# Windowed attention and two dense layers: the loads of later attention heads issued by SyncE, between the weight loads, instead of by GpSimd

## The chip, the cores and the metric

The kernel runs on one core of a Trainium2 chip. What is measured is the device time of one execution in microseconds (us); lower is better. The core's engines run side by side, each through its own list of instructions in order: TensorE (PE in the profile), VectorE (DVE), ScalarE (ACT), GpSimd (POOL) and SyncE (SP). They wait for each other by semaphores. DMA transfers are issued by an engine's list (here SyncE and GpSimd) and then run by themselves; a semaphore is raised when one has landed.

## The reference

Two batches of 8 heads, 768 positions, head dimension 64. Attention is limited to the last 128 positions and the first 4 (sinks). Its output, 1536 tokens of 512 features, goes through two dense layers of width 2048.

```python
scores = scale * np.matmul(q, k.transpose(0, 1, 3, 2))
keep = is_sink | in_window                 # pos < 4, or 0 <= rel < 128
scores = np.where(keep, scores, -1000000000.0)
a = np.exp(scores - np.max(scores, axis=-1, keepdims=True))
a = a / (np.sum(a, axis=-1, keepdims=True) + 1e-09)
x = np.matmul(a, v)                        # then heads side by side: 1536 x 512

h = x @ w_in                               # layer 1: 512 -> 2048
g = np.where(h >= 1, h, np.where(h <= -1, 0.0, (h + 1) ** 2 / 4))
x = g @ w_out                              # 2048 -> 512

h = x @ w_in2                              # layer 2
g = np.where(h > 0.0, h, np.exp(np.minimum(h, 0.0)) - 1.0)
y = g @ w_out2
```

All inputs are float32.

## The kernel before

The tokens are cut into six chunks of 256. Layer 1 runs over them one by one, and beside layer 1 of a chunk the kernel computes the attention of the next chunk; only chunk 0's attention stands alone, at the start (`first_...`). Layer 2 then runs over three chunks of 512 tokens. To keep precision, every operand of the dense layers is split in two parts, `_hi` (a rounding that TensorE multiplies fast, made by ScalarE) and `_lo` (the rest, made by VectorE by a subtraction), and each product is three matmuls (lines 507 to 509 and 522 to 524). The keys and queries of a head are split likewise (`split_head`, lines 593, 594 on ScalarE, 782, 783 on VectorE).

A layer's chunk has 16 steps t, one per 128 of the 2048 hidden features. A step of TensorE is `hidden(t)` (12 matmuls into `h_ps`), `outward(t - 2)` (12 matmuls) and, beside them, parts of the attention of the next chunk: `attention_plan` puts the scores of heads 0 to 7 at steps 2, 3, 5, 6, 8, 9, 11, 12, a head's exponentials one step later, its transposes two steps later, and a pair's values three steps after its second head. A head h > 0 is split at the head of its own step (`before_layer`), head 0 between two chunks.

The weights come in groups of 512 KB, 16 for a layer (`load_weights`, line 290). During layer 1 of chunk 0 they are split too: groups 0 to 2 before it, group 3 + t at the end of step t (`splits_first`; ScalarE line 644, VectorE line 840). A weight group is loaded into one of six buffers: groups 0 to 4 take the first five, group 5 + n takes buffer n mod 6. A load therefore waits (line 284) until the group that had its buffer has been split: group 5 until group 0 has, ..., group 9 until group 4 has, group 10 takes a new buffer once the first attention is over, group 11 waits for group 5, ..., group 15 for group 9. SyncE issues these loads in a fixed order written out by hand (lines 292 to 318), then the stores of the result.

The loads for the attention of chunks 1 to 5 are issued by GpSimd (`load_head`, `load_values`, lines 370 to 388, called from line 394 on). The keys of a head (260 KB, `ks`) and its queries (128 KB, `qs`) go into one of two buffers, by the parity of the head; a load waits until the head before the last has been split by VectorE (`qk_lo_ready`). Heads 0 and 1 of chunk 1 wait for the first chunk's scores instead. The values of a pair of heads (192 KB and 36 KB, `vals`) go into one of two buffers, and wait until the pair before the last has been used (`attn_ready`; for the first two, `first_attn`). GpSimd also builds the masks at the start and copies the mask of each chunk (line 409).

What sets the order of the work is thus the list of each engine; an engine that waits in its list holds up all that stands behind it.

Of the kernel before, what the change touches and what calls it, by code (L numbers as in the profile page):

```python
# [30 lines left out]
B, HEADS, SEQ, HD = 2, 8, 768, 64  # L31
# [3 lines left out]
NC = TOK // CT  # L35
# [4 lines left out]
PAIRS = HEADS // 2  # L40
# [5 lines left out]
NW = 2 * GROUPS  # L46
# [35 lines left out]
def build(nc, qk_first, v_first, q_t, k_t, v_w, v_s, w_in, w_out, ident_d, out, n_sink, window):  # L82
# [6 lines left out]
    KS = 2 * LOW + 2 * NS  # L89

    with ExitStack() as ctx:
# [6 lines left out]
        def sem(name):  # L98
            return ctx.enter_context(nc.semaphore(name))
# [24 lines left out]
        qs, ks = sb0("qs", [P, 2, CT]), sb0("ks", [P, 2, QB * SW])  # L124
# [3 lines left out]
        vs = vals[:, 0:6 * P].rearrange("p (s b d) -> p s b d", s=2, b=3)  # L128
        vsink = vals[:, 6 * P:8 * P].rearrange("p (s d) -> p s d", s=2)
# [21 lines left out]
        first_scores, first_max, first_neg_max, first_exp = sem("first_scores"), sem("first_max"), sem("first_neg_max"), sem("first_exp")  # L151
        first_sum, first_inv, first_probs, first_probs_t = sem("first_sum"), sem("first_inv"), sem("first_probs"), sem("first_probs_t")
        first_copied, first_attn = sem("first_copied"), sem("first_attn")
        qk_loaded = [sem(f"qk_loaded{n}") for n in range(4)]
        v_loaded = [sem("v_loaded0"), sem("v_loaded1")]
# [46 lines left out]
        def heads_before(c, h=0):  # L202
            return (c - 1) * HEADS + h

        def pairs_before(c, p=0):
            return (c - 1) * PAIRS + p
# [64 lines left out]
        @block.sync  # L271
        def _(sp):
            def load_first_head_pair(p):
                sp.dma_start(first_qk[p][0], qk_first[p, :, 0, :]).then_inc(first_qk_loaded[p], 16)
                sp.dma_start(first_qk[p][1], qk_first[p, :, 1, :]).then_inc(first_qk_loaded[p], 16)

            def load_first_values(p):
                sp.dma_start(first_v[p], v_first[p]).then_inc(first_v_loaded[p], 16)

            def load_weights(i):  # L280
                n = order[i]
                layer, m = n // NW, n % NW
                if splits_until_free(i) > 0:
                    sp.wait_ge(w_lo_ready, splits_until_free(i))
                if i < NW and place[i] >= FEW:
                    sp.wait_ge(first_attn, PAIRS)
                if i >= NW:
                    sp.wait_ge(attn_ready, pairs_before(NC))
                src = (w_in if m % 2 == 0 else w_out)[layer, m // 2]
                sp.dma_start(raw_buffer(i), src).then_inc(raw_loaded[place[i]], 16)  # L290

            load_first_head_pair(0)
            load_first_head_pair(1)
            sp.dma_start(ident[:, :], ident_d).then_inc(ident_loaded, 16)
            load_first_values(0)
            load_first_head_pair(2)
            load_first_values(1)
            load_weights(0)
            load_first_head_pair(3)
            load_first_values(2)  # L300
            load_first_values(3)
            load_weights(1)
            load_weights(2)
            load_weights(3)
            load_weights(4)
            load_weights(5)
            load_weights(6)
            load_weights(7)
            load_weights(8)
            load_weights(9)  # L310
            load_weights(10)
            load_weights(11)
            load_weights(12)
            load_weights(13)
            load_weights(14)
            load_weights(15)
            for i in range(NW, 2 * NW):
                load_weights(i)
            with sp.Fori(0, NC1) as c:
                for m in range(KT):  # L320

                    sp.wait_ge(y_written, NC * len(y_ps) + (c * KT + (m + 1)))
                    sp.dma_start(out[:, m, bass.ts(c, CT1)], chunk(c, 1)[:, m, :]).then_inc(stored, 16)
            sp.wait_ge(stored, 16 * NC1 * KT)


        @block.gpsimd
        def _(pool):
            steps = [0]

            def step(ins):
                steps[0] += 1
                ins.then_inc(mask_step, 1)
                pool.wait_ge(mask_step, steps[0])

            def keep_where(view, base, pattern, channel):
                step(nc.gpsimd.affine_select(out=view, in_=view, compare_op=ALU.is_ge, fill=MASKED / SCALE,
                                             base=base, pattern=pattern, channel_multiplier=channel))

            def build_mask(m, kind):  # L340

                step(nc.gpsimd.memset(m, 0.0))
                for j in range(QB):
                    start = j * MW + NS
                    prev, own = m[:, start:start + P], m[:, start + P:start + WIN]
                    if kind == 0 and j == 0:
                        step(nc.gpsimd.memset(prev, MASKED / SCALE))
                    else:

                        keep_where(prev, window - 1 - P, [[1, P]], -1)  # L350

                    keep_where(own, 0, [[-1, P]], 1)
                    if window < P:
                        keep_where(own, window - 1, [[1, P]], -1)
                    if kind == 0:
                        step(nc.gpsimd.memset((own if j == 0 else prev)[:, 0:NS], MASKED / SCALE))

            def build_first_mask(m):

                step(nc.gpsimd.memset(m, 0.0))  # L360
                own0, prev1, own1 = (m[:, n * P:(n + 1) * P] for n in range(3))
                for own in (own0, own1):
                    keep_where(own, 0, [[-1, P]], 1)
                    if window < P:
                        keep_where(own, window - 1, [[1, P]], -1)
                keep_where(prev1, window - 1 - P, [[1, P]], -1)
                for sinks in (own0, prev1):
                    step(nc.gpsimd.memset(sinks[:, 0:NS], 0.0))

            def load_head(c, h):  # L370
                if isinstance(c, int) and c == 1 and h < 2:

                    pool.wait_ge(first_scores, h + 2)
                else:
                    pool.wait_ge(qk_lo_ready, heads_before(c, h) - 1)
                for to, src in zip((ks[:, h % 2, :], qs[:, h % 2, :]), (k_t, q_t)):
                    pool.dma_start(to, src[bass.ds(heads_before(c, h), 1)].rearrange("o p n -> (o p) n")).then_inc(qk_loaded[h % 4], 16)  # L377

            def load_values(c, p):
                s = p % 2  # L380
                if isinstance(c, int) and c == 1 and p < 2:
                    pool.wait_ge(first_attn, PAIRS - 1)
                else:
                    pool.wait_ge(attn_ready, pairs_before(c, p) - 1)
                n = pairs_before(c, p)
                pool.dma_start(vs[:, s, :, :].rearrange("p b d -> p (b d)"),
                             v_w[bass.ds(n, 1)].rearrange("o p n -> (o p) n")).then_inc(v_loaded[s], 16)
                pool.dma_start(vsink[0:KS, s, :], v_s[bass.ds(n, 1)].rearrange("o p n -> (o p) n")).then_inc(v_loaded[s], 16)

            build_first_mask(mask[:, 0:SEEN])  # L390
            pool.sem_inc(mask_ready, 1)
            build_mask(masks[:, 0, :], 0)
            build_mask(masks[:, 1, :], 1)
            load_head(1, 0)
            load_head(1, 1)
            pool.wait_ge(first_max, HEADS * QB)
            nc.gpsimd.tensor_copy(mask[:, :], masks[:, 1, :]).then_inc(mask_ready, 1)
            load_values(1, 0)
            load_values(1, 1)
            for h in range(2, HEADS):  # L400
                load_head(1, h)
                if h > 2 * 2 and h % 2 == 1:
                    load_values(1, h // 2)
            with pool.Fori(2, NC) as c:
                load_head(c, 0)
                load_head(c, 1)
                pool.wait_ge(max_done, heads_before(c) * QB)
                kind = (c % CPB + (CPB - 1)) // CPB
                nc.gpsimd.tensor_copy(mask[:, :], masks[:, bass.ds(kind, 1), :].rearrange("p o n -> p (o n)")).then_inc(mask_ready, 1)
                for p in range(PAIRS):  # L410
                    if p > 0:
                        load_head(c, 2 * p)
                        load_head(c, 2 * p + 1)
                    load_values(c, p)


        @block.tensor
# [563 lines left out]
```

## Time and profile before

| | us |
|---|---|
| median of 3 runs (lowest, highest) | 656.87 (655.11, 657.06) |
| the profiled execution | 657.06 |
| its span, first to last instruction | 655.4 |
| TensorE busy | 635.3 |
| VectorE busy | 378.3 |
| ScalarE busy | 350.0 |
| GpSimd busy | 74.3 |

The profile records one execution. The span is shorter than the time by 1.7 us, which lie before the first and after the last instruction. Matmuls overlap in TensorE's pipeline, so its busy time says how much of the span it has something under way, not how fast it works. A wait in a list of waits is the idle time of an engine ahead of an instruction, with the engine or transfer that ended it. The time of a DMA transfer "to landing" is counted from its issue.

### The profile page before, as it was taken

How to read it: one execution, taken by the hardware profiler on the slowest of the kernel's cores; microseconds unless marked ns; L12 is line 12 of the kernel's file. 1: busy time of each engine (PE TensorE's matmuls, PEld its weight loads, DVE VectorE, ACT ScalarE, POOL GpSimd, SP SyncE). 2: the span in 40 equal slices, each digit the busy share in tenths (PEclk: the TensorE clock that was granted, in tenths of full speed). 3: DMA queues.
4: the chain of work that ended last, by engine and by line, in shares of the span. 5: the costliest groups of instructions: out<-in, count | busy, mean ns of one | idle time of the engine just before them, and what ended most of it. 6: DMA issues, size and time to landing. Idle time of an engine off the chain costs nothing.

```text
span 655.4 us, 12200 instructions
## 1 busy us (share of the span) xinstructions
PE 635.3 (97%) x4164; PEld 562.6 (86%) x4164; DVE 378.3 (58%) x994; ACT 350.0 (53%) x830; POOL 74.3 (11%) x147
## 2 busy tenths in 40 slices
PE   5789999999999999999999999999999999999997
PEld 3688889999999999999999988888888888888886
DVE  6799968886886788588757863322332222322221
ACT  5687756665665666566656563333443333533333
POOL 4111221320322122123000000000000000000000
PEclk9799999999999999999999999999999999999999
DMA  7674212320322222122044600000100000100001
GB/s 277 188 221 143 69 39 85 91 77 24 100 65 63 62 66 86 38 77 86 25 161 161 188 7 0 1 0 1 49 16 0 0 0 0 64 0 0 0 0 64
DMA packets 15275, 42.48 MB, mean 65 GB/s; under 512 B 2852, under 2 KB 4536, under 8 KB 15248
## 3 DMA queue, kind: packets, MB, share of 16 engines
q0 software_dynamic: 7040, 20.57, 10.7%
q1 hardware_dynamic: 8208, 21.56, 9.8%
q8 instruction: 15, 0.25, 0.2%
q14 instruction: 12, 0.10, 0.0%
HBM read 38.98 MB, written 3.15 MB: 64 GB/s over the span
## 4 chain that ended last, share of the span: by engine, by line
PE 88%; DVE 9%; ACT 1%; issue 1%; DMA 0%; ACTq 0%; SPq 0%; DVEq 0%
PE h_ps L507 13%; PE h_ps L509 13%; PE h_ps L508 13%; PE y_ps L522 10%; PE y_ps L524 9%; PE y_ps L523 9%; PE s_ps L524 3%; PE s_ps L523 3%; PE s_ps L522 3%; PE o_ps L490 3%; PE t_ps L470 2%; DVE wout_lo L840 1%; PE s_ps L461 1%; PE s_ps L460 1%; DVE win_lo L840 1%
## 5 line engine op out<-in xcount | busy, mean ns | idle before, releaser
L507 PE MATMUL h_ps<-x_hi,win_hi 128*128 128x256 f32 (+1 forms) x576 | 186.9, 324 | 0.4
L509 PE MATMUL h_ps<-x_hi,win_lo 128*128 128x256 f32 (+1 forms) x576 | 185.2, 321 | 0.0
L508 PE MATMUL h_ps<-x_lo,win_hi 128*128 128x256 f32 (+1 forms) x576 | 184.2, 320 | 0.0
L522 PE MATMUL y_ps<-g_hi,wout_hi 128*128 128x256 f32 (+1 forms) x480 | 147.1, 306 | 1.7 <-DVE g_lo L853 1.6
L524 PE MATMUL y_ps<-g_hi,wout_lo 128*128 128x256 f32 (+1 forms) x480 | 146.4, 305 | 0.0
L523 PE MATMUL y_ps<-g_lo,wout_hi 128*128 128x256 f32 (+1 forms) x480 | 145.9, 304 | 0.0
L870 DVE SCALAR_TENSOR_TENSOR g_full<-g_full,h_ps 128x512 f32<-128x512 f32 x48 | 33.1, 690 | 156.6 <-ACT g_full L675 156.6
L507 PEld LDWEIGHTS h_ps<-x_hi,win_hi 128*128 128x128 f32 x576 | 108.7, 189 | 10.6 <-DVE g_full L866 1.0
L508 PEld LDWEIGHTS h_ps<-x_lo,win_hi 128*128 128x128 f32 x576 | 109.2, 190 | 9.4
L509 PEld LDWEIGHTS h_ps<-x_hi,win_lo 128*128 128x128 f32 x576 | 108.9, 189 | 8.3
L662 ACT CAST g_hi<-g_full 128x256 fp32r<-128x256 f32 (+1 forms) x144 | 68.5, 476 | 68.6 <-DVE g_full L870 34.2
L853 DVE TENSOR_TENSOR g_lo<-g_full,g_hi 128x256 fp32r<-128x256 f32 (+1 forms) x144 | 73.7, 512 | 51.5 <-ACT g_hi L662 50.8
L522 PEld LDWEIGHTS y_ps<-g_hi,wout_hi 128*128 128x128 f32 x480 | 90.1, 188 | 7.8 <-issue 2.0
L523 PEld LDWEIGHTS y_ps<-g_lo,wout_hi 128*128 128x128 f32 x480 | 90.6, 189 | 4.7
L524 PEld LDWEIGHTS y_ps<-g_hi,wout_lo 128*128 128x128 f32 x480 | 90.4, 188 | 4.2
L673 ACT ACTIVATE ramp<-h_ps 128x512 f32<-128x512 f32 x48 | 28.8, 600 | 121.9 <-PE h_ps L509 121.8
L603 ACT ACTIVATE probs<-s_ps,small 128x260 f32<-128x260 f32 x80 | 37.4, 471 | 27.2 <-DVE small L798 27.1
L670 ACT ACTIVATE ramp<-h_ps,small 128x256 f32<-128x256 f32 x96 | 45.6, 475 | 7.7 <-PE h_ps L509 7.7
L864 DVE SCALAR_TENSOR_TENSOR g_full<-ramp 128x256 f32<-128x256 f32 x96 | 40.4, 421 | 10.6 <-ACT ramp L670 10.6
L377 POOL DMA_DIRECT2D ks<-in_k x40 | 22.1, 552 | 215.2 <-DVE q_parts L783 213.4
L866 DVE TENSOR_TENSOR g_full<-g_full,h_ps 128x256 f32<-128x256 f32 x96 | 40.4, 421 | 3.3
L524 PE MATMUL s_ps<-g_hi,wout_lo 128*128 128x512 f32 x96 | 38.3, 399 | 0.0
(109 smaller groups left out, 819.2 us busy)
## 6 DMA issues: line engine op xcount, KB each, us to landing
ks<-in_k POOLq DMA_DIRECT2D x40, 260.0 KB, 3.0
raw<-in_w_in SPq DMA_DIRECT2D x11, 512.0 KB, 4.3
raw<-in_w_out SPq DMA_DIRECT2D x11, 512.0 KB, 3.5
qs<-in_q POOLq DMA_DIRECT2D x40, 128.0 KB, 2.8
vals<-in_v POOLq DMA_DIRECT2D x20, 192.0 KB, 3.1
out_y<-xy SPq DMA_DIRECT2D x12, 256.0 KB, 2.1
xy<-in_w_in SPq DMA_DIRECT2D x5, 512.0 KB, 4.9
xy<-in_w_out SPq DMA_DIRECT2D x5, 512.0 KB, 4.0
```

The costliest lines, as they stand in the source:

```text
L507: pe.matmul(o, win_hi[:, k, f], x_hi[:, k, :], start=(k == 0), stop=False)
L508: pe.matmul(o, win_hi[:, k, f], x_lo[:, k, :], start=False, stop=False)
L509: last = pe.matmul(o, win_lo[:, k, f], x_hi[:, k, :], start=False, stop=(k == KT - 1))
L522: pe.matmul(o, wout_hi[:, t, cols], g_hi[:, t % GR, :], start=begin, stop=False, skip_group_check=True)
L523: pe.matmul(o, wout_hi[:, t, cols], g_lo[:, t % GR, :], start=False, stop=False, skip_group_check=True)
L524: last = pe.matmul(o, wout_lo[:, t, cols], g_hi[:, t % GR, :], start=False, stop=(t == FT - 1), skip_group_check=True)
L603: nc.scalar.activation(probs[:, j, hh * SW:(hh + 1) * SW], s_ps[j][:, 0:SW], ACT.Exp, bias=top[:, hh, j:j + 1], accum_out=total[:, hh, j:j ...
L662: nc.scalar.copy(g_hi[:, t % GR, :], g_full[:, t % 2, :]).then_inc(g_hi_ready, 1)
L670: nc.scalar.activation(ramp[:, t % 2, :], h, ACT.Relu, bias=half[:, 0:1], scale=0.5).then_inc(ramp_ready, 1)
L853: nc.vector.tensor_tensor(g_lo[:, t % GR, :], g_full[:, t % 2, :], g_hi[:, t % GR, :].bitcast(F32), ALU.subtract).then_inc(g_lo_ready, 1)
L864: nc.vector.scalar_tensor_tensor(g, r, 1.0, r, ALU.min, ALU.mult).then_inc(bent_ready, 1)
L866: nc.vector.tensor_tensor(g, g, h, ALU.max).then_inc(g_ready, 1)
```

## The change

The functions `load_head` and `load_values` move from GpSimd to SyncE, unchanged but for the engine that waits and issues. On SyncE the loads of chunk 1 are put between the weight loads by hand: heads 0 and 1 and the first values behind group 4, head 2 behind group 6, head 3 and the second values behind group 8, and heads 4 to 7 with their values behind group 15, the last of layer 1. Chunks 2 to 5 follow in a loop, then the weights of layer 2 as before. GpSimd keeps the masks and their copies. 120 transfers (40 of keys, 40 of queries, 40 for values) change the engine that issues them; none is added or removed, and their sizes are the same.

```diff
--- before.py
+++ after.py
@@ def _(sp):
+            def load_head(c, h):
+                if isinstance(c, int) and c == 1 and h < 2:
+                    sp.wait_ge(first_scores, h + 2)
+                else:
+                    sp.wait_ge(qk_lo_ready, heads_before(c, h) - 1)
+                for to, src in zip((ks[:, h % 2, :], qs[:, h % 2, :]), (k_t, q_t)):
+                    sp.dma_start(to, src[bass.ds(heads_before(c, h), 1)].rearrange("o p n -> (o p) n")).then_inc(qk_loaded[h % 4], 16)
+
+            def load_values(c, p):
+                s = p % 2
+                if isinstance(c, int) and c == 1 and p < 2:
+                    sp.wait_ge(first_attn, PAIRS - 1)
+                else:
+                    sp.wait_ge(attn_ready, pairs_before(c, p) - 1)
...
+
+            def load_pair(c, p):
+                load_head(c, 2 * p)
+                load_head(c, 2 * p + 1)
+                load_values(c, p)
...
             load_weights(4)
+            load_head(1, 0)
+            load_head(1, 1)
+            load_values(1, 0)
             load_weights(5)
             load_weights(6)
+            load_head(1, 2)
             load_weights(7)
             load_weights(8)
+            load_head(1, 3)
+            load_values(1, 1)
             load_weights(9)
-            load_weights(10)
...
-            load_weights(15)
+            for i in range(10, NW):
+                load_weights(i)
+            load_pair(1, 2)
+            load_pair(1, 3)
+            with sp.Fori(2, NC) as c:
+                for p in range(PAIRS):
+                    load_pair(c, p)
             for i in range(NW, 2 * NW):
                 load_weights(i)
@@ def _(pool):
-            def load_head(c, h):
...
             build_mask(masks[:, 1, :], 1)
-            load_head(1, 0)
-            load_head(1, 1)
             pool.wait_ge(first_max, HEADS * QB)
             nc.gpsimd.tensor_copy(mask[:, :], masks[:, 1, :]).then_inc(mask_ready, 1)
-            load_values(1, 0)
-            load_values(1, 1)
-            for h in range(2, HEADS):
-                load_head(1, h)
-                if h > 2 * 2 and h % 2 == 1:
-                    load_values(1, h // 2)
             with pool.Fori(2, NC) as c:
-                load_head(c, 0)
-                load_head(c, 1)
+
                 pool.wait_ge(max_done, heads_before(c) * QB)
                 kind = (c % CPB + (CPB - 1)) // CPB
                 nc.gpsimd.tensor_copy(mask[:, :], masks[:, bass.ds(kind, 1), :].rearrange("p o n -> p (o n)")).then_inc(mask_ready, 1)
-                for p in range(PAIRS):
-                    if p > 0:
-                        load_head(c, 2 * p)
-                        load_head(c, 2 * p + 1)
-                    load_values(c, p)
```

## Rows read from the trace of the kernel before

**Rows 1.** The page: busy us (share of span) xinstructions.

```profile
PE 635.3 (97%) x4164; PEld 562.6 (86%) x4164; DVE 378.3 (58%) x994; ACT 350.0 (53%) x830; POOL 74.3 (11%) x147
```

**Rows 2.** Stretches: length; busy us PE, PEld, DVE, ACT, POOL; granted clock; DMA share, GB/s.

```profile
60.00:84.50 24.50, 22.73 (x186) 20.95 (x187) 23.60 (x66) 18.36 (x49) 7.21 (x12) 1.00 0.26 76
...
96.00:150.00 54.00, 53.96 (x460) 52.23 (x459) 43.05 (x139) 34.82 (x101) 13.64 (x25) 1.00 0.27 78
```

**Rows 3.** Waits: who waited for whom, us in total, times, longest.

```profile
POOL ks L377 <- DVE q_parts L783: 213.4, 38, 12.7
...
PE o_ps L450 <- issue: 1.9, 1, 1.9
```

**Rows 4.** ScalarE in order of time: start us, length, line, operation.

```profile
26.11 0.63 ACT L593 CAST k_hi<-ks 128x520 fp32r<-128x520 f32 x1
...
33.03 1.04 ACT L644 CAST wout_hi<-raw 128x1024 fp32r<-128x1024 f32 x1
...
51.69 1.05 ACT L644 CAST wout_hi<-xy 128x1024 fp32r<-128x1024 f32 x1
...
57.78 0.65 ACT L593 CAST k_hi<-ks 128x520 fp32r<-128x520 f32 x1
```

**Rows 5.** GpSimd in order of time, its loads; in brackets the wait.

```profile
22.04 0.54 POOL L386 DMA_DIRECT2D vals<-in_v  x1 [6.24 <-PE o_ps L450]
...
28.51 0.54 POOL L377 DMA_DIRECT2D ks<-in_k  x1 [4.33 <-DVE q_parts L783]
...
38.04 0.62 POOL L377 DMA_DIRECT2D ks<-in_k  x1 [8.46 <-DVE q_parts L783]
...
46.58 0.54 POOL L377 DMA_DIRECT2D ks<-in_k  x1 [7.40 <-DVE q_parts L783]
```

**Rows 6.** SyncE in order of time, weight groups 9, 10 and 15.

```profile
33.48 0.34 SPq L290 DMA_DIRECT2D xy<-in_w_out  x1
...
33.86 0.43 SPq L290 DMA_DIRECT2D xy<-in_w_in  x1
...
55.91 0.34 SPq L290 DMA_DIRECT2D xy<-in_w_out  x1
```

**Rows 7.** DMA issues at 33.8 and 56 us, and the start's: KB, us to landing.

```profile
xy<-in_w_out SPq DMA_DIRECT2D x1, 512.0 KB, 4.0
...
xy<-in_w_in SPq DMA_DIRECT2D x1, 512.0 KB, 4.9
...
xy<-in_w_out SPq DMA_DIRECT2D x1, 512.0 KB, 3.3
...
ks<-in_qk_first SPq DMA_DIRECT2D x4, 128.0 KB, 2.4
```

**Rows 8.** VectorE in order of time, heads 0 and 4.

```profile
27.08 0.70 DVE L782 TENSOR_TENSOR k_lo<-ks,k_hi 128x520 fp32r<-128x520 f32 x1 [0.41 <-ACT q_parts L594]
...
59.08 0.69 DVE L782 TENSOR_TENSOR k_lo<-ks,k_hi 128x520 fp32r<-128x520 f32 x1
```

**Rows 9.** TensorE in order of time, near 60 and 86 us.

```profile
60.27 0.39 PE L460 MATMUL s_ps<-k_hi,q_parts 128*128 128x260 f32 x1 [0.59 <-DVE q_parts L783]
...
85.58 0.36 PE L522 MATMUL y_ps<-g_hi,wout_hi 128*128 128x256 f32 x1 [0.60 <-DVE g_lo L853]
```

**Rows 10.** VectorE's line 782, all heads: ns min/median/max.

```profile
L782 DVE TENSOR_TENSOR k_lo<-ks,k_hi x40: 692/700/703, 27.1 to 319.2; 128x520 fp32r<-128x520 f32 x40
```

**Rows 11.** Stretches around the fall of the clock, as in rows 2.

```profile
14.42:21.24 6.82, 3.48 (x32) 2.46 (x30) 5.43 (x19) 5.67 (x16) 0.62 (x1) 1.00 0.74 273
...
21.24:28.07 6.83, 5.82 (x31) 4.44 (x28) 4.13 (x10) 3.48 (x7) 2.14 (x4) 0.50 0.72 221
...
55.38:62.20 6.82, 6.00 (x49) 5.52 (x48) 6.64 (x18) 6.70 (x16) 1.07 (x2) 1.00 0.35 105
```

**Rows 12.** Chain of waits near 27 and 92 us: start us, us, what.

```profile
26.75 0.21 PE h_ps L507
...
92.11 0.12 PE y_ps L522
```

More of the change, by code:

```diff
@@ L278, in load_first_values @@
                 sp.dma_start(first_v[p], v_first[p]).then_inc(first_v_loaded[p], 16)
+            def load_head(c, h):
[11 more added lines that the diff above has]
+                    sp.wait_ge(attn_ready, pairs_before(c, p) - 1)
+                n = pairs_before(c, p)
+                sp.dma_start(vs[:, s, :, :].rearrange("p b d -> p (b d)"),
+                             v_w[bass.ds(n, 1)].rearrange("o p n -> (o p) n")).then_inc(v_loaded[s], 16)
+                sp.dma_start(vsink[0:KS, s, :], v_s[bass.ds(n, 1)].rearrange("o p n -> (o p) n")).then_inc(v_loaded[s], 16)
+            def load_pair(c, p):
+                load_head(c, 2 * p)
+                load_head(c, 2 * p + 1)
+                load_values(c, p)
             def load_weights(i):
@@ L305, in _ @@
             load_weights(4)
+            load_head(1, 0)
+            load_head(1, 1)
+            load_values(1, 0)
             load_weights(5)
             load_weights(6)
+            load_head(1, 2)
             load_weights(7)
             load_weights(8)
+            load_head(1, 3)
+            load_values(1, 1)
             load_weights(9)
-            load_weights(10)
[L312 to L315, printed above, removed]
-            load_weights(15)
+            for i in range(10, NW):
[5 more added lines that the diff above has]
+                    load_pair(c, p)
             for i in range(NW, 2 * NW):
@@ L368, in build_first_mask @@
                     step(nc.gpsimd.memset(sinks[:, 0:NS], 0.0))
-            def load_head(c, h):
[L371 to L388, printed above, removed]
             build_first_mask(mask[:, 0:SEEN])
```

## The prediction

> **What bounds the kernel now.** I read the page first, then the busy time by stretches, then who waits for whom. On the page TensorE is busy for 635.3 us of the span of 655.4 us [rows 1]. The stretches divide this in two. From about 96 us on TensorE has no holes (53.96 us busy of 54.00); the attention of the later chunks and both layers run at its pace, and what another engine or queue does there costs nothing as long as it keeps up. In chunk 0 (25 to 86 us) it is VectorE that has none: 23.60 us busy of 24.50 between 60.00 and 84.50 us, TensorE 22.73 [rows 2]. That chunk splits one weight group per step beside its attention. So a stop of VectorE there moves everything behind it, and later stages have no spare time in which to catch up.
>
> The waits say who needed the loads that are moved. GpSimd stood 213.4 us at the head loads, waiting for VectorE to free a head's buffer [rows 3]; in the whole list of waits nobody waits for one of these loads to land. They are hidden everywhere today, so the move can only gain if GpSimd's issuing harms somebody, and can lose wherever SyncE's order is later than GpSimd's.
>
> **The change, part by part.** I work through SyncE's new order with the times at which each wait ends today.
>
> Heads 0 and 1 of chunk 1: issued behind weight group 4, at about 9.5 and 11 us, behind 2.5 MB of weights (6.4 us at the rate worked out below), and head 0 is taken by ScalarE at 26.11 us [rows 4]. Nothing.
>
> Weight group 5 now stands behind the first values, whose wait ends at 22.04 us [rows 5]: it is issued at 23.0 us and, at the 4.9 us that is the longest landing used below, there at 27.9 us; ScalarE casts it at 33.03 us [rows 4]. Group 6 follows at 23.4 us and is cast later still. Group 7 stands behind head 2, whose wait ends at 28.51 us [rows 5]; two issues of 0.45 us put it at 29.4 us, and it is cast two steps after group 5; a step of chunk 0 is some 60/16 = 3.8 us. Hidden.
>
> Group 9 (33.48 us) now stands behind head 3, whose wait ends at 38.04 us [rows 5, 6], and behind two issues for it and two for values: 38.04 + 4 x 0.45 = 39.9 us. Groups 10 and 11 follow at 40.3 and 40.8 us, group 12 is where it was. Head 3, these values and the four groups are 2.66 MB in a row; at the rate worked out below (512 KB in 1.28 us) that is 6.7 us, over by 47 us, and group 9, the first of the groups, is cast at 51.69 us [rows 4]. Hidden.
>
> Head 4 is the one that isn't. Today its wait (head 2 split) ends at 46.58 us [rows 5] and GpSimd issues it at once, 11.2 us before ScalarE takes it at 57.78 us [rows 4]. After the change it stands behind weight groups 10 to 15, and group 15 waits until group 9 has been split: it is issued at 55.91 us [rows 6]. Head 4's keys are then issued at 55.91 + 0.34 + 0.04 = 56.3 us and its queries at 56.75 us. Now the landing. Group 15 lands 3.3 us after its issue [rows 7], at 59.2 us. Groups 9 and 10, issued back to back at 33.48 and 33.86 us, landed 4.0 and 4.9 us later [rows 6, 7], at 37.48 and 38.76 us: the second 512 KB took 1.28 us behind the first. So 260 KB of keys and 128 KB of queries behind group 15 take 0.65 + 0.32 us, and head 4 has landed at 60.2 us.
>
> There the Trainium skill has a rule (DMA: Bandwidth & Descriptors, "Queues, rings and completion order"): one issuing engine's transfers are consumed in ring order, while a GpSimd row is taken in turn with it, packet by packet. The landings of groups 9 and 10 [rows 7] agree with it: the later one has its 1.28 us to itself. Were SyncE's transfers shared out instead, head 4 could land near 59.1 us and the cost below would be some 1.1 us smaller.
>
> From landing to VectorE: ScalarE casts keys and queries, and VectorE started on head 0's keys 0.97 us after ScalarE did (26.11 to 27.08 us) [rows 4, 8]. So VectorE can start head 4 at 60.2 + 0.97 = 61.2 us. Today it starts at 59.08 us, straight from group 10's split with no idle time [rows 8]. It now stands still for 2.1 us. ScalarE's other work of the step (the cast of g and the ramp of step 8) comes behind the head's casts in its order and is late by as much. TensorE waited for VectorE's q_parts at 60.27 us already (0.59 us idle), and at 85.58 us for g_lo [rows 9]: it has no work in hand that could fill the hole, and VectorE no idle time before 85.6 us that could take it back. The 2.1 us go through to the end.
>
> What I take the 2.1 us from, and its bounds: at best, head 4's queries land like the 128 KB loads of the start, 2.4 us from their issue [rows 7], at 59.15 us; VectorE starts at 60.1 us and loses 1.0 us. At worst they take what group 10 took, 4.9 us, and land at 61.65 us: a loss of 3.5 us. The middle way is nearest to what follows a 512 KB transfer in this queue, so I keep 2.1.
>
> Head 5 is issued at 57.2 us, lands by 61.2 (0.97 us behind head 4) and is cast a step (3.8 us) later than head 4. The values of pair 2 follow at 58 us and are used three steps on. From here SyncE has caught up with VectorE: heads 6 and 7 and all of chunks 2 to 5 wait for the same semaphores in the same order as on GpSimd, with the same lead (a head is freed three steps before its successor is split). An issue takes 0.43 us on SyncE instead of 0.54 us on GpSimd; nobody waits for either. The second layer's weights waited for the last attention anyway.
>
> What GpSimd loses: 120 issues. What remains is the mask copy, whose waits don't change. If these issues disturbed VectorE, its instructions would differ in length where they meet. The split of the keys takes 692 to 703 ns over all 40 heads [rows 10]. I take nothing for it; what it would be worth if the harm lay in the gaps between them is rival C.
>
> Sum, against the profiled execution: 657.06 + 2.1 = 659.2 us (span 657.5). The median of the runs shown, 656.87, lies 0.2 us below that execution: 659.0. I take 659.1. That is 0.33% slower; I count 0.3% (2.0 us) as what a measurement of this kernel can tell from no change, so this forecast sits right on that bound.
>
> **Rivals.**
> A. The stall takes the clock with it. In chunk 0's beginning TensorE, busy 3.48 of 6.82 us, was followed by 6.83 us at a granted clock of 0.50 (1.2 GHz) [rows 11]. With the stall it would stand idle 2.1 + 0.6 us in one piece, in a stretch of which it now works 6.00 of 6.82 us. In the slow stretch a matmul follows the last after 0.21 us, at full clock after 0.12 us [rows 12]; 6.8 us at that pace do 3.9 us of work where 6.0 are due: 2.1 us more, 661.3 us. For it: what TensorE does there, some 3.9 us of 6.8, would be near the 3.48 that it did before the fall. Against it: it is still more, and no later stretch of the trace has fallen.
> B. Head 4 is hidden after all. This needs its landing by 58.1 us (59.08 - 0.97), that is its issue by about 55 us, and hence group 9's split or group 15's issue at least 1 us earlier against VectorE's work on group 10. Both hang on VectorE's one order, so only a much shorter latency than SyncE's rows show could do it. Then 656.9 us, no slower.
> C. GpSimd's issues cost the others something that the lengths of instructions hide. VectorE's gaps are 0.90 us of 24.50 [rows 2], 2.2 us over the 60 us of chunk 0, and TensorE has one wait of 1.9 us, in the first 25 us where weights and heads 0 and 1 share the queues, for which the profile names no releaser [rows 3]. If all of both went, 657.06 + 2.1 - 2.2 - 1.9 = 655.1 us, and 654.0 with the stall at its lower bound. Against it: GpSimd has 12 instructions in those 24.50 us, VectorE 66 [rows 2], so most of its gaps can't be GpSimd's.
> D. A second late load in chunk 0: group 9 to 12's burst, late only if the transfers ran at under half the rate of groups 9 and 10; some 3 us more, 662 us.
>
> **How the numbers follow.** Forecast (stall of 1.0 to 3.5 us and nothing else) 0.62; A 0.13; B 0.12; C 0.09; D 0.04. The forecast's own range is 657.9 to 660.6 us, and the bound of 0.3% lies at 658.8: I give 0.37 of its 0.62 to slower, 0.25 to no change. Slower: 0.37 + 0.13 + 0.04 = 0.54. Same: 0.25 + 0.12 + 0.02 of C = 0.39. Faster: 0.07 of C. The runs of before spread by 2 us, so the range takes B in at its lower end and A at its upper: 656.3 to 661.6 us.
>
> **What would show it.** In the profile after: head 4's load on SyncE's queue right behind weight group 15 at about 56 us; ScalarE's cast of head 4's keys idle about 2.4 us with the load of ks or qs as releaser, the first wait on a head load anywhere; VectorE idle about 2.1 us before k_lo; TensorE idle 2.7 us at the scores of head 4; every later event late by the same amount; from 96 us on no change of pace. Wrong if no such wait stands in ScalarE's list, or if k_lo starts where it did; rival A if the granted clock falls again near 62 to 70 us; C if instructions or gaps of VectorE before 56 us are shorter.

## The result, and the profile after

| | median us | lowest, highest | runs |
|---|---|---|---|
| before | 655.11 | 653.98, 657.30 | 13 |
| after | 657.25 | 656.72, 661.80 | 13 |

The changed kernel is slower: its time is 1.0052 times that of the kernel before, 95% interval 1.0035 to 1.0069. The medians lie 2.1 us apart. The forecast was 659.1 us (range 656.3 to 661.6), slower by 2.1 us. The ratio compares means, which lie further apart, because part of the changed kernel's runs lie 2 to 5 us over its median. The base was 1.8 us too high: ten more runs brought the median of the kernel before down from 656.87 to 655.11 us.

That the medians lie just as far apart as forecast is partly luck. More runs are on record: 38 in all of the changed kernel, with a median of 658.92 us, and 66 of the kernel before, taken beside the experiments, with a median of 655.07. These medians lie 3.9 us apart, and the lowest runs, 656.68 and 653.83 us, 2.9 us. (One more run of the kernel before, of 690 us at a mean clock of 0.85, was slow in another way and is left out everywhere.)

The profiled execution took 661.64 us, with a span of 659.9 us. The page: TensorE does the same 4164 matmuls, GpSimd has nothing left but its masks, and the granted clock has a dip in the fourth and fifth slices (49 to 82 us) that the kernel before doesn't have.

```profile
PE 637.5 (97%) x4164; PEld 565.3 (86%) x4164; DVE 378.4 (57%) x994; ACT 349.8 (53%) x830; POOL 9.3 (1%) x27
...
PEclk9798899999999999999999999999999999999999
...
q1 hardware_dynamic: 24288, 42.13, 20.4%
```

The stretches that answer to [rows 2]: between 60.00 and 84.50 us VectorE is busy for 20.20 us where it was for 23.60; from 96 us on TensorE has as few holes as before.

```profile
60.00:84.50 24.50, 20.23 (x147) 18.82 (x148) 20.20 (x54) 17.99 (x46) 0.00 (x0) 0.86 0.30 88
...
96.00:150.00 54.00, 53.96 (x460) 51.96 (x457) 43.65 (x140) 35.23 (x102) 0.63 (x1) 1.00 0.28 78
```

The waits up to 90 us. The first line has no counterpart in the kernel before: ScalarE waits for a head load to land. The second, TensorE's waits for VectorE's split of the queries, was 4.3 us in seven waits before, the longest 1.1.

```profile
ACT k_hi L591 <- DMA qs<-in_q: 3.3, 1, 3.3
...
PE s_ps L458 <- DVE q_parts L781: 6.8, 6, 3.6
```

SyncE in order of time, around weight group 15 (first line; answers to the last of [rows 6]), and head 4's keys and queries behind it, head 5's keys behind these. Under it the same two loads of head 4 with their time to landing in us.

```profile
56.11 0.34 SPq L315 DMA_DIRECT2D xy<-in_w_out  x1
...
56.50 0.43 SPq L287 DMA_DIRECT2D ks<-in_k  x1
...
56.97 0.43 SPq L287 DMA_DIRECT2D qs<-in_q  x1
...
57.45 0.43 SPq L287 DMA_DIRECT2D ks<-in_k  x1
```

```profile
ks<-in_k SPq DMA_DIRECT2D x1, 260.0 KB, 3.8
...
qs<-in_q SPq DMA_DIRECT2D x1, 128.0 KB, 4.4
```

The queries, issued at 56.97 us, have landed at 61.37. ScalarE, VectorE and TensorE in order of time, in brackets the idle time before; they answer to the last lines of [rows 4], [rows 8] and the first of [rows 9]:

```profile
57.04 1.07 ACT L642 CAST win_hi<-xy 128x1024 fp32r<-128x1024 f32 x1
...
61.38 0.62 ACT L591 CAST k_hi<-ks 128x520 fp32r<-128x520 f32 x1 [3.27 <-DMA qs<-in_q]
```

```profile
58.14 1.23 DVE L838 TENSOR_TENSOR win_lo<-xy,win_hi 128x1024 fp32r<-128x1024 f32 x1
...
62.34 0.70 DVE L780 TENSOR_TENSOR k_lo<-ks,k_hi 128x520 fp32r<-128x520 f32 x1 [2.97 <-ACT q_parts L592]
```

```profile
63.53 0.59 PE L458 MATMUL s_ps<-k_hi,q_parts 128*128 128x260 f32 x1 [3.63 <-DVE q_parts L781]
```

ScalarE stands for 3.27 us until the queries are there, VectorE for 2.97 us until ScalarE has cast them, TensorE for 3.63 us until VectorE has split them. Then the clock (columns as in rows 2; the granted clock is the third number from the end):

```profile
56.60:63.40 6.80, 3.07 (x25) 2.59 (x23) 3.78 (x8) 3.54 (x9) 0.00 (x0) 0.94 0.71 228
...
63.40:70.20 6.80, 6.67 (x34) 6.39 (x36) 6.51 (x20) 4.39 (x13) 0.00 (x0) 0.56 0.27 66
...
70.20:77.00 6.80, 6.80 (x63) 6.63 (x60) 5.44 (x16) 5.12 (x12) 0.00 (x0) 1.00 0.27 89
```

TensorE was busy for 3.07 of 6.80 us, and for most of the next 6.80 us its clock is 1.2 GHz (0.56 in the mean), after which it has 2.4 GHz again. Cut finer, the trace shows the low clock from 62.6 to 69.4 us.

**Where the 4.5 us between the two profiled executions are.** VectorE takes head 4's keys at 59.08 us before and could have at 62.34 - 2.97 = 59.37 us after: 0.3 us come from the start. The stop is 2.97 us. From that instruction (k_lo) to the end there are 655.4 - 59.08 = 596.3 us before and 659.9 - 62.34 = 597.6 us after: 1.2 us, which I put down to the time at the low clock; the table below bears this out. Together 4.5 us. This split (start, stop, rest) is used for every kernel below.

### The profile page after: what moved, and what is told of

Same layout as the page of the kernel before. It is cut to its first block, busy times and chain, and to the rows that moved or that the text cites. A ratio compares the mean times of both kernels' runs of the same rounds, so it can differ in the third digit from the quotient of the medians.

```text
span 659.9 us, 12209 instructions
## 1 busy us (share of the span) xinstructions
PE 637.5 (97%) x4164; PEld 565.3 (86%) x4164; DVE 378.4 (57%) x994; ACT 349.8 (53%) x830; POOL 9.3 (1%) x27
## 2 busy tenths in 40 slices
DMA packets 24314, 42.47 MB, mean 64 GB/s; under 512 B 2752, under 2 KB 13536, under 8 KB 24288
## 3 DMA queue, kind: packets, MB, share of 16 engines
q1 hardware_dynamic: 24288, 42.13, 20.4%
## 4 chain that ended last, share of the span: by engine, by line
PE 89%; DVE 7%; ACT 2%; issue 1%; DMA 1%; SPq 0%; ACTq 0%; DVEq 0%
PE h_ps L505 13%; PE h_ps L507 13%; PE h_ps L506 13%; PE y_ps L520 10%; PE y_ps L522 9%; PE y_ps L521 9%; PE s_ps L520 3%; PE s_ps L522 3%; PE s_ps L521 3%; PE o_ps L488 3%; PE t_ps L468 2%; PE s_ps L458 1%; PE s_ps L459 1%; DVE wout_lo L838 1%; PE o_ps L490 1%
## 5 line engine op out<-in xcount | busy, mean ns | idle before, releaser
L505 PE MATMUL h_ps<-x_hi,win_hi 128*128 128x256 f32 (+1 forms) x576 | 188.8, 328 | 0.4
L862 DVE SCALAR_TENSOR_TENSOR g_full<-ramp 128x256 f32<-128x256 f32 x96 | 40.3, 420 | 10.7 <-ACT ramp L668 10.7
L520 PE MATMUL s_ps<-g_hi,wout_hi 128*128 128x512 f32 x96 | 38.3, 399 | 0.0
```

The costliest lines, as they stand in the source:

```text
L505: pe.matmul(o, win_hi[:, k, f], x_hi[:, k, :], start=(k == 0), stop=False)
L520: pe.matmul(o, wout_hi[:, t, cols], g_hi[:, t % GR, :], start=begin, stop=False, skip_group_check=True)
L862: nc.vector.scalar_tensor_tensor(g, r, 1.0, r, ALU.min, ALU.mult).then_inc(bent_ready, 1)
```

## The experiments

The line numbers differ by a few from kernel to kernel. The table has the split of all of them in us; k_lo is VectorE's first instruction on head 4, the split of its keys.

All columns but the last two are from each kernel's profile, the last two from its own runs. "Low clock" is how long TensorE was granted 1.2 GHz after the stop; low clocks in the start, before 30 us, are not in it.

| kernel | VectorE's stop before head 4 | k_lo starts | span | k_lo to the end | low clock | lowest run | median |
|---|---|---|---|---|---|---|---|
| before | 0 | 59.08 | 655.4 | 596.3 | 0 | 653.98 | 655.11 |
| after | 2.97 | 62.34 | 659.9 | 597.6 | 6.8 | 656.72 | 657.25 |
| head 4 early | 0 | 56.95 | 653.1 | 596.2 | 0 | 653.81 | 654.59 |
| head 4 ahead of group 15 | 0.72 | 59.63 | 655.8 | 596.2 | 0 | 654.63 | 655.07 |
| head 5 held | 2.39 | 58.31 | 654.8 | 596.5 | 3.4 | 656.50 | 658.80 |
| GpSimd late | 2.75 | 59.91 | 656.4 | 596.5 | 3.4 | 656.81 | 657.83 |
| GpSimd later | 4.66 | 64.26 | 661.1 | 596.8 | 6.8 | 659.71 | 662.49 |
| after, stall filled | 2.66 | 60.51 | 656.7 | 596.2 | 0 | 657.63 | 658.22 |
| head 4 early, start filled | 0 | 56.02 | 652.2 | 596.2 | 0 | 653.81 | 654.54 |

Where the clock doesn't fall behind the stop, the rest takes 596.2 or 596.3 us, whatever the stop was: nothing takes a stop up. With 3.4 us of low clock it takes 0.3 us more, with 6.8 us 0.5 (GpSimd later) and 1.2 us (after) more. In GpSimd later TensorE still stood idle, without work to slow down, for 2.4 of the 6.8 us, in after for 0.9.

**1. Undo the lateness alone.** The changed kernel with head 4 issued earlier in SyncE's order, and with it head 5 and the values of their pair ahead of group 15; all loads stay on SyncE.

```diff
-            for i in range(10, NW):
-                load_weights(i)
-            load_pair(1, 2)
+            for i in range(10, 14):
+                load_weights(i)
+            load_head(1, 4)
+            load_weights(14)
+            load_head(1, 5)
+            load_values(1, 2)
+            load_weights(15)
             load_pair(1, 3)
```

> The changed kernel with one thing moved in SyncE's order: head 4 is issued behind weight group 13 (about 46.6 us) and head 5 with the values of pair 2 behind group 14 (about 51.9 us), instead of all behind group 15. Theory (the loss is head 4's late landing, and the clock that falls after it): ScalarE's wait for head 4 and VectorE's stop of 3 us are gone, no second fall of the clock, the time is that of the kernel before within 1 us (654 to 657), in every run. Rival 1 (issuing 120 transfers from SyncE, or their queue, costs time by itself): it stays 2 to 3 us above the kernel before. Rival 2 (GpSimd's issues cost something, hidden in the changed kernel by the stall): it ends over 1 us below the kernel before.

Measured: 654.59 us median of 12 runs (653.81 to 657.22), beside 655.04 for the kernel before; ratio 1.0004, interval 0.9986 to 1.0021. VectorE in order of time goes from the split of group 10 straight to head 4's keys, as in the kernel before:

```profile
55.80 1.23 DVE L842 TENSOR_TENSOR win_lo<-xy,win_hi 128x1024 fp32r<-128x1024 f32 x1
...
56.95 0.69 DVE L784 TENSOR_TENSOR k_lo<-ks,k_hi 128x520 fp32r<-128x520 f32 x1
```

Both rivals fall: 120 transfers issued by SyncE instead of GpSimd neither cost nor gain anything that can be measured (within 0.2%). The whole loss of the change is in the place of the loads behind group 15, of which only head 4's were waited for. A kernel in which SyncE issues the 96 transfers of chunks 2 to 5 alone gave no time, so they were not measured by themselves. In this profile head 4's k_lo starts 2.1 us earlier than in that of before; its low clock in the start was 3.4 us long instead of 6.8.

**2. The lateness alone, on GpSimd.** The kernel before with one wait more.

```diff
             for h in range(2, HEADS):
+                if h == 4:
+                    pool.wait_ge(w_lo_ready, 10)
                 load_head(1, h)
```

> The kernel before, with one wait more on GpSimd: head 4 is issued only when weight group 9 has been split, the moment at which SyncE reaches it in the changed kernel; queue and engine are the old ones. Theory (it is the moment of issue, not the engine or queue): issue at 55.9 us, queries issued at 56.5, landed 3.6 to 4.1 us later at 60.1 to 60.6 us, VectorE stops for 2.0 to 2.5 us, time 2 to 2.5 us above the kernel before, in some runs 2 to 4 us more with a second fall of the clock. Rival (the loss needs SyncE's queue): within 0.5 us of the kernel before.

Measured: 657.83 us median of 10 runs (656.81 to 660.51), ratio 1.0049 (1.0030 to 1.0068), the same as the change's. GpSimd's issue of head 4's keys and VectorE's start on them:

```profile
54.16 0.56 POOL L377 DMA_DIRECT2D ks<-in_k  x1 [16.98 <-DVE wout_lo L842]
```

```profile
59.91 0.70 DVE L784 TENSOR_TENSOR k_lo<-ks,k_hi 128x520 fp32r<-128x520 f32 x1 [2.75 <-ACT q_parts L596]
```

So neither SyncE nor its queue is needed for the loss: a late issue beside group 15's transfer makes it. The stop is 0.25 us longer than the 2.5 us at the upper end of the expectation, and the queries took 4.2 us to land beside group 15's 512 KB, where 3.6 to 4.1 were expected.

**3. Ahead of group 15.** The changed kernel with head 4 issued at the same moment but before the weight group.

```diff
-            for i in range(10, NW):
+            for i in range(10, 15):
                 load_weights(i)
-            load_pair(1, 2)
+            sp.wait_ge(w_lo_ready, splits_until_free(15))
+            load_head(1, 4)
+            load_weights(15)
+            load_head(1, 5)
+            load_values(1, 2)
```

> The changed kernel, with head 4 issued at the same moment (group 9 split) but ahead of weight group 15, head 5 still behind it. Theory (part of the delay is group 15's 512 KB and head 5's keys in the same queue): queries issued at 56.5 to 56.6 us land 2.6 to 3.0 us later, at 59.3, VectorE stops for about 1 us instead of 3; time 1 us above the kernel before, no second fall of the clock. Rival (place in the queue doesn't matter, the transfers share it evenly): it lands at 60.5 to 61.4 us as in the changed kernel and the time is the same as there.

Measured: 655.07 us median (654.63 to 658.35), ratio 1.0013 (0.9994 to 1.0033). The queries now land 2.6 us after their issue instead of 4.4; VectorE's stop shrinks to 0.72 us:

```profile
qs<-in_q SPq DMA_DIRECT2D x1, 128.0 KB, 2.6
```

```profile
59.63 0.70 DVE L784 TENSOR_TENSOR k_lo<-ks,k_hi 128x520 fp32r<-128x520 f32 x1 [0.72 <-ACT q_parts L596]
```

The landing accounts for 1.8 us of the 2.25 that the stop shrinks by; the rest is the issue, 0.5 us sooner after group 9's split. The place in one engine's queue matters: the rival expected the landing and the time of the changed kernel, and neither came.

**4. Head 5 held back.** The changed kernel, head 5 and the values of pair 2 not issued before head 4 has landed.

```diff
-            load_pair(1, 2)
+            load_head(1, 4)
+            sp.wait_ge(qk_loaded[0], 64)
+            load_head(1, 5)
+            load_values(1, 2)
```

> The changed kernel, with head 5 and the values of pair 2 held on SyncE until head 4 has landed. Theory (the term that I had too small, head 4's landing at 61.4 us instead of 60.2 + 0.2, is contention with head 5's keys and queries, issued right behind): head 4's queries land 3.4 to 3.7 us after their issue instead of 4.4, VectorE stops for 2.0 to 2.3 us instead of 2.97, the lowest time is 0.7 to 1.0 us under the changed kernel's 656.7. Rival (head 4's own rows or the queue behind a 512 KB transfer take that long): it lands 4.4 us after the issue as before, stop of 3.0 us, same time.

Measured: the queries land 3.8 us after their issue instead of 4.4, and VectorE stops for 2.39 us instead of 2.97:

```profile
ks<-in_k SPq DMA_DIRECT2D x1, 260.0 KB, 3.7
...
qs<-in_q SPq DMA_DIRECT2D x1, 128.0 KB, 3.8
```

```profile
58.31 0.70 DVE L783 TENSOR_TENSOR k_lo<-ks,k_hi 128x520 fp32r<-128x520 f32 x1 [2.39 <-ACT q_parts L595]
```

Both numbers moved the way of the theory and lie just outside what it expected (3.4 to 3.7 and 2.0 to 2.3 us). One profile of each kernel is thin evidence for 0.6 us: the profile of experiment 6, in which these loads are issued in the same order as in the changed kernel, has the queries landing after 4.1 us, not 4.4. And in experiment 3, where group 15's 512 KB and head 5 were issued right behind head 4's queries, these landed after 2.6 us, which is the median of all 40 loads of queries in the changed kernel. So it is not shown that what is issued behind delays a load. In the times it doesn't appear: the lowest of six runs is 656.50 us, 0.2 us under the changed kernel's and not 0.7 to 1.0; the median, 658.80, is above it. Six runs don't resolve half a microsecond against the clock's spread. What is left of the landing time (3.8 against the 3.4 of the prediction's sum) is not explained.

**5. A larger dose.** As experiment 2, with `w_lo_ready` at 11.

> The kernel before, head 4 on GpSimd made to wait for group 10's split (about 59.2 us) instead of group 9's (55.9). Theory (landing time decides, one for one): the issue is 3.3 us later than in the run with GpSimd late, so is the landing, and VectorE's stop grows from 2.75 to about 6 us; the time without a fall of the clock is 6 us above the kernel before, 660 to 661 us, and the clock falls in most runs, to 662 to 664 us. Rival (there is slack that takes up part of a stall): less than 5 us above.

Measured: 659.71 to 662.79 us in four runs, ratio 1.0084 (1.0054 to 1.0114). VectorE's stop is 4.66 us, not 6:

```profile
59.90 0.54 POOL L377 DMA_DIRECT2D ks<-in_k  x1 [20.28 <-DVE win_lo L842]
```

```profile
64.26 0.70 DVE L784 TENSOR_TENSOR k_lo<-ks,k_hi 128x520 fp32r<-128x520 f32 x1 [4.66 <-ACT q_parts L596]
```

Group 15, issued at 56.35 us, has landed after 3.4 us, before head 4's keys are issued, and the queries take 2.9 us instead of 4.2. The expectation treated the landing time as fixed and missed by that. Nothing takes the stop up: k_lo to the end is 596.8 us, 0.5 more than before, with 6.8 us of low clock in it. The lowest run is 5.8 us above the lowest of the kernel before beside it (653.91), so the rival of slack (less than 5 us) falls too; that this is 1.1 us more than the stop is not explained.

**6. The stall filled.** The changed kernel with 24 matmuls more, whose results the scores overwrite.

```diff
             def scores(c, h):
+                if isinstance(c, int) and c == 1 and h == 4:
+                    pe.wait_ge(exp_done, heads_before(c, h) * QB)
+                    for n in range(24):
+                        pe.matmul(s_ps[0][:, 0:CT], win_hi[:, n % KT, 0:P], x_hi[:, n % KT, :], start=True, stop=True)
                 pe.wait_ge(qk_lo_ready, heads_before(c, h) + 1)
```

> The changed kernel, with 24 matmuls of 256 columns added on TensorE while it waits for head 4's split (results overwritten by the scores that follow; the output doesn't change). They take 24 x 0.12 = 2.9 us of a wait of 3.6 us. Theory (the second fall of the clock comes from TensorE's idle time in the stall): no run has a granted clock under 0.995, all times near 657.2, none at 660 to 662. Rival (the fall has another cause): as in the changed kernel, some 4 in 10 runs at 659 to 662 us with a clock of 0.99.

TensorE in order of time, the added matmuls and the scores of head 4; and the two stretches of 6.8 us around them:

```profile
58.11 3.12 PE L456 MATMUL s_ps<-x_hi,win_hi 128*128 128x256 f32 x24
...
61.70 0.39 PE L462 MATMUL s_ps<-k_hi,q_parts 128*128 128x260 f32 x1 [0.47 <-DVE q_parts L785]
```

```profile
54.60:61.40 6.80, 6.40 (x53) 5.98 (x51) 4.02 (x10) 3.85 (x9) 0.00 (x0) 1.00 0.70 230
...
61.40:68.20 6.80, 6.16 (x51) 5.51 (x52) 6.51 (x19) 5.84 (x15) 0.00 (x0) 1.00 0.25 67
```

TensorE is busy for 6.40 us where the changed kernel had 3.07, and the clock stays at 2.4 GHz; VectorE's stop of 2.66 us is still there, and k_lo to the end is 596.2 us, as short as in any kernel. So in this profile the low clock went with TensorE's idle time in the stall.

The other kernels with a stall that nothing fills show a low clock behind it in their profiles too, though shorter in two of them (the column "low clock" above). TensorE had stood idle for 3.08 us (head 5 held), 3.44 (GpSimd late), 3.63 (after) and 5.32 us (GpSimd later); it has no low clock there after 0.47 us (stall filled), 0.59 (before, head 4 early) or 1.41 us (head 4 ahead of group 15). Here is GpSimd late, up to the fall and behind it:

```profile
55.60:62.40 6.80, 3.36 (x29) 3.05 (x29) 3.97 (x8) 3.71 (x10) 2.83 (x6) 1.00 0.56 204
62.40:65.80 3.40, 3.40 (x19) 3.40 (x18) 3.29 (x9) 2.96 (x9) 0.01 (x1) 0.52 0.39 117
```

The runs without a profile have only their mean clock. A profile with 3.4 us of low clock in all has a mean of 0.997, one with 6.8 us 0.995, one with 13.6 us 0.990. All 38 runs of the changed kernel have 0.997 or less, 13 of them 0.991 or less; of the 66 runs of the kernel before 31 have 0.999 or 1.000, and one has less than 0.992. The low clock of the start alone would thus leave about half of the runs at 0.999 or more. Of the six runs with the stall filled three have 1.000 and none less than 0.992. So some fall of the clock belongs to the unfilled stall in all the changed kernel's runs, or nearly all, and what differs from run to run is its length and the low clock in the start. The expectation of 0.995 in every run of this kernel missed, by low clocks in the start, which this kernel doesn't touch. The times are no better: the lowest is 657.63 us, 0.9 above the changed kernel's, and one run (659.88 us) is above 659. Why, the profile doesn't show; it stays open.

**7 to 9. The clock in the start.** The kernels above with ten runs or more all spread over 3 us or more, with or without the change. Head 4 early, with 16 matmuls added in the first attention:

```diff
             def first_values(p):
                 pe.wait_ge(first_v_loaded[p], 16)
-                pe.wait_ge(first_copied, 2 * (p + 1))
                 if p >= IN_FLIGHT:
                     pe.wait_ge(x_lo_ready, p - IN_FLIGHT + 1)
+                for n in range((0, 6, 8, 2)[p]):
+                    pe.matmul(flight[p % IN_FLIGHT][1][:, CT:CT + P], ident[:, :], ident[:, :], start=True, stop=True)
+                pe.wait_ge(first_copied, 2 * (p + 1))
```

Experiment 7, expected:

> The kernel with head 4 early, and in the first attention 16 matmuls of 128 columns added on TensorE where it waits for ScalarE's copies (at 15.7, 18.8 and 23.6 us; results are overwritten, the output doesn't change). Theory (the 3 us of spread among the runs of every kernel, 654 to 657, is the clock's fall after TensorE's idle time in the first 21 us): granted clock 1.00 in all runs, all times at or below 654.1. If so this version is faster than both kernels, median against median, by 0.5 to 1 us. Rival (the spread has another cause, or 128-column matmuls delay the start): the same spread, or 1 us added.

Experiment 8, the kernel before with the same matmuls:

> The kernel before with the 16 matmuls in the first attention alone, loads on GpSimd. Theory (the gain of the version with the filled start comes from the clock in the start, and nothing from where the loads are issued): all runs at 653.8 to 655.3 us, granted clock 0.997 or more, the same as that version within 0.5 us. Rival (moving the loads away from GpSimd gives part of that gain): 0.5 to 1 us above it.

Experiment 9, the kernel of experiment 7 once more, on the chip of experiment 8:

> The version with head 4 early and the filled start once more, on the same chip as the one above. Theory: 653.8 to 655.3 us, equal to it within 0.5 us. Rival (GpSimd's issues cost time): 0.5 to 1 us below it.

| | median | lowest, highest | median of before, same chip | ratio, interval |
|---|---|---|---|---|
| head 4 early, start filled | 654.54 | 653.81, 655.24 | 656.29 | 0.9973 (0.9961 to 0.9985) |
| the same again | 654.46 | 653.93, 655.43 | 654.24 | 0.9994 (0.9982 to 1.0006) |
| before, start filled | 654.46 | 653.95, 655.06 | 654.24 | 0.9989 (0.9977 to 1.0001) |

One stretch of the start, in the kernel of experiment 7 and in the kernel before:

```profile
13.00:25.80 12.80, 11.83 (x100) 9.71 (x97) 10.08 (x30) 9.82 (x27) 0.62 (x1) 0.98 0.63 223
```

```profile
13.00:25.80 12.80, 8.45 (x55) 5.16 (x51) 9.41 (x30) 9.20 (x26) 2.76 (x5) 0.82 0.76 268
```

TensorE is busy for 11.83 us instead of 8.45, at a mean clock of 0.98 instead of 0.82. No run of the three series is above 655.5 us, while those of the kernel before beside them reach 657.4: the upper half of the spread does come from the clock in the start. Not each low clock there costs time: this profile of experiment 7, of a run of 654.00 us, has 3.4 us of it, from 10.2 us on. The expectation that all would be at or below 654.1 us missed: half the runs lie at 654.4 to 655.4 us, nearly all of these at a clock of 1.00, and what makes that step was not tried. It is faster than both kernels only against runs in which the clock falls in the start: the ratio is 0.9973 in one series and not different from 1 in the other. With loads on GpSimd or on SyncE it is the same (654.46 and 654.46), a second sign that who issues them is worth nothing.

## Why the prediction was right or wrong

- **What bounds the kernel.** Right. The stop of VectorE in chunk 0 arrives at the end in full in every kernel: k_lo to the end is 596.2 or 596.3 us where the clock doesn't fall behind it, whatever the stop was. That later stages have no time in which to catch up was the base of the sum.
- **Weight groups 5 to 12, heads 0 to 3: nothing.** Right: in the profile after no wait on a DMA appears up to 90 us but this one and the first one of the start, which both kernels have.
- **Head 4 late.** Right, in place and cause: group 15 at 56.11 us (55.91 predicted), keys at 56.50 (56.3), queries at 56.97 (56.75). Experiment 1 takes the loss away by moving this head, experiment 2 makes it without the change.
- **The size of the stop.** Predicted 2.1 us within 1.0 to 3.5; measured 2.97. The step that was too small is the landing, 61.37 us instead of 60.2. Of these 1.17 us 0.2 are the start, 0.2 group 15, which landed 3.5 us after its issue and not 3.3, and 0.75 the queries: "260 KB of keys and 128 KB of queries behind group 15 take 0.65 + 0.32 us" holds for the keys (0.7), but the queries came 1.07 us behind them. Why the queries took so long stays open. Experiment 4 points to the loads issued behind them (0.6 us sooner with these held back), experiment 3 against it (2.6 us with group 15 and head 5 right behind). The Trainium skill's ring order (DMA: Bandwidth & Descriptors, "Queues, rings and completion order") agrees with experiment 3, where the place in the queue was worth 1.8 us of landing time, but the prediction's sum over what is ahead came out 1 us short here.
- **Rival A, the clock.** Happened in the profiled execution, and was given 0.13, which was too little: by the mean clocks some low clock comes with the stall in all the changed kernel's runs, or nearly all. "Stall and nothing else" is not what happened. Where the low clock was as long as the rival had it, 6.8 us, its price was 1.2 us, and 0.5 in experiment 5, not 2.1. The rival priced the matmuls that TensorE would not get done; but VectorE bounds this stage, busy for 6.51 of 6.80 us from 63.40 us on, so TensorE's slowness counts only in part. Where it was 3.4 us long, it cost 0.3 us. It goes with the stall: experiment 6, and its absence in experiments 1 and 3.
- **Rival B (hidden).** Did not happen. With the landing as measured it would need head 4 issued 3 us sooner; ahead of group 15 a stop of 0.72 us is left (experiment 3: ratio 1.0013, interval across 1).
- **Rival C (GpSimd's issues cost something).** Wrong: experiments 1 and 8 against 9.
- **Rival D (a second late load).** Did not happen.
- **Later chunks.** Right: TensorE is busy for 53.96 us of 54.00 in both kernels.
- **The number.** 657.25 us lies inside the range, and 1.85 us under the forecast. The base is 1.8 us of this. The sum had the stop 0.9 us too small; but the median of before lies 1.1 us above its lowest run, that of the changed kernel 0.5 us above its own, and the distance of the medians shrinks by the difference. That the two errors nearly cancel is luck. The lowest runs are the cleaner comparison: 2.9 us apart over all runs on record, with a stop of 2.97 us.
- **Base.** Three runs of the kernel before were not enough for its median: it can lie anywhere between 654.2 and 656.3 us, as its own series show, by where the clock falls in the start.

## What to carry to other kernels

When loads move to another engine's list, go through the new order with the times at which its waits end today and compare each issue, plus its landing, with the moment of first use. Add up the landing from what is ahead in the queue and leave a margin: here this sum was 1 us short. A load behind another's wait inherits that wait. A transfer that nobody waits for has nothing to gain and its whole cover to lose. A stop of the engine that bounds a stage adds in full if later stages are bound by another engine, and an idle TensorE may add the clock to it.

## What the runs showed of the hardware

- A stall of 3.6 us in a stage that TensorE doesn't bound brought its clock down to 1.2 GHz (granted clock 0.56 from 63.40 to 70.20 us); with the same stall filled by matmuls it stayed at 2.4 GHz. In the start the runs of a kernel spread over some 3 us; with TensorE's gaps there filled, over 1.6 us (653.81 to 655.43 us in 36 runs).
- A clock at 1.2 GHz costs little in a stage that another engine bounds: 0.3 us for 3.4 us of it, 0.5 and 1.2 us for 6.8.
- A load's time to landing depends on what surrounds it in the queues: 128 KB of queries, right behind 260 KB of keys each time, took 2.6 us ahead of a 512 KB load, 2.9 us on GpSimd's queue when it had landed, 3.8 us right behind it, 4.2 us on GpSimd's queue beside it, and 4.4 us (4.1 in experiment 6) right behind it with 616 KB more following. Each is one transfer in one profile.
- The whole kernel made 15,275 packets with these loads on GpSimd and 24,314 with them on SyncE, for the same 42.5 MB, and the DMA engines' share of time was the same (10.7 + 9.8% and 20.4%): more and smaller packets took no more of them.
